# A linear-attention recurrence with two expert layers: chunks of 128 tokens cut into sub-chunks of 64 on 64x64 matmul tiles

## The reference, cut to what matters

```
cur  = (u * k_t) outer v_t
y_t  = r_t @ (state + cur)
state = w[:, None] * state + k_t outer v_t
```

```
logits = x @ phi                       # 3072 x 32 slots, 8 experts of 4 slots
d = softmax of logits over tokens;  slot_input = d.T @ x
slot_out = relu(slot_input @ w1[e]) @ w2[e]      # 384 -> 1024 -> 384 per expert
c = softmax of logits over slots;   x2 = c @ slot_out
out = relu(x2 @ w_in) ** 2 @ w_out     # 384 -> 2048 -> 384
```

## Time and profile before

| what | us |
|---|---|
| time, median of 3 runs (465.07 to 466.24) | 465.87 |
| profiled execution, span from first to last instruction | 464.3 |
| first output of a unit ends | 23.08 |
| last output of a unit (unit 23) ends | 178.30 |
| first matmul of the experts | 190.56 |
| first matmul of the last stage | 228.05 |

### The profile page before, as it was taken

One profiled execution on the slowest core, in us unless ns is written; L12 is line 12 of the kernel. 1 busy time (PEld: TensorE's weight loads), 2 busy tenths in 40 slices (PEclk: granted clock), 3 DMA queues, 4 the chain that ended last, 5 costly groups with the idle time before them and its releaser, 6 DMA issues.

```text
span 464.3 us, 8783 instructions
## 1 busy us (share of the span) xinstructions
PE 405.0 (87%) x3096; PEld 349.0 (75%) x3096; DVE 331.9 (71%) x439; ACT 174.4 (38%) x312; POOL 153.1 (33%) x111
## 2 busy tenths in 40 slices
PE   0856968778787889999679999999999999999997
PEld 0544857657676766235279999999999999999997
DVE  8599999999999994611596565565556556556553
ACT  2011313123031314012535555555555555555552
POOL 6578878898888850110550000000000000000000
PEclk9957999999998989899889999999999999999999
DMA  6966667667666769999600010001001001001001
GB/s 174 243 195 193 202 206 218 183 201 231 194 196 203 225 238 316 373 373 403 212 0 1 1 68 2 1 1 68 0 0 68 0 0 68 0 0 68 1 0 68
DMA packets 31844, 60.30 MB, mean 130 GB/s; under 512 B 2640, under 2 KB 25296, under 8 KB 31440
## 3 DMA queue, kind: packets, MB, share of 16 engines
q1 hardware_dynamic: 31824, 60.02, 40.9%
HBM read 55.30 MB, written 4.72 MB: 129 GB/s over the span
## 4 chain that ended last, share of the span: by engine, by line
PE 61%; DVE 14%; POOL 10%; issue 5%; DVEq 1%; ACT 1%; POOLq 0%; ACTq 0%
PE out_ps L1081 43%; POOL scores L413 8%; PE h_ps L1059 5%; DVE scores L667 4%; DVE queries L644 4%; PE wide L997 3%; PE wide L1022 2%; PE score_ps L865 2%; DVE bonus L662 1%; DVE state L680 1%; PE y_ps L890 1%; POOL ruk L402 1%; POOL ruk L405 1%; PE wide L948 1%; DVE keys L638 1%
## 5 line engine op out<-in xcount | busy, mean ns | idle before, releaser
L1081 PE MATMUL out_ps<-w_hi,act_hi 128*128 128x384 f32 x384 | 130.5, 340 | 5.2 <-DVE act_lo L819 4.0
L1081 PE MATMUL out_ps<-w_hi,act_lo 128*128 128x384 f32 x384 | 131.0, 341 | 0.0
L1081 PE MATMUL out_ps<-w_lo,act_hi 128*128 128x384 f32 x384 | 130.5, 340 | 0.0
L814 DVE TENSOR_TENSOR act<-relu_h 128x512 f32<-128x512 f32 x96 | 68.2, 711 | 78.3 <-ACT relu_h L576 78.3
L576 ACT ACTIVATE relu_h<-h_ps 128x512 f32<-128x512 f32 x96 | 57.3, 597 | 100.6 <-PE h_ps L1059 97.9
L865 PE MATMUL score_ps<-queries,keys 112*128 112x256 f32 x192 | 60.5, 454 | 29.7 <-DVE queries L644 29.7
L413 POOL TENSOR_TENSOR scores<-ident,bonus 128x1024 f32<-128x1024 f32 x24 | 74.4, 3101 | 23.2 <-DVE bonus L662 23.2
L1081 PEld LDWEIGHTS out_ps<-w_hi,act_hi 128*128 128x128 f32 x384 | 72.7, 189 | 6.2 <-ACT act_hi L579 3.3
L1081 PEld LDWEIGHTS out_ps<-w_lo,act_hi 128*128 128x128 f32 x384 | 72.9, 190 | 3.8
L1081 PEld LDWEIGHTS out_ps<-w_hi,act_lo 128*128 128x128 f32 x384 | 72.5, 189 | 0.0
L819 DVE TENSOR_TENSOR act_lo<-act,act_hi 128x512 fp32r<-128x512 f32 x96 | 68.4, 713 | 4.6 <-ACT act_hi L579 1.0
(11 more groups left out here) (145 smaller groups left out, 369.1 us busy)
## 6 DMA issues: line engine op xcount, KB each, us to landing
rkv<-in_rkv_n SPq DMA_DIRECT2D x24, 576.0 KB, 4.6
rk<-in_rk_t SPq DMA_DIRECT2D x48, 192.0 KB, 3.2
w_sb<-in_w SPq DMA_DIRECT2D x24, 384.0 KB, 5.1
w_room<-in_w SPq DMA_DIRECT2D x4, 1536.0 KB, 11.1
out_dram<-y_sb SPq DMA_DIRECT2D x5, 768.0 KB, 3.5
w_x<-in_w SPq DMA_DIRECT2D x2, 1536.0 KB, 14.0
w_w<-in_w SPq DMA_DIRECT2D x4, 768.0 KB, 11.5
w_in_sb<-in_w_in SPq DMA_DIRECT2D x3, 1024.0 KB, 13.0
```

Of the source, the lines that this page charges most:

```text
L814: nc.vector.tensor_tensor(act[f % 2][:, :], relu_h[f % 2][:, :], relu_h[f % 2][:, :], ALU.mult).then_inc(act_done, 1)
L1081: last = nc.tensor.matmul(out_ps[t][:, 0:DM], a[f % 4][:, tok], w[:, f], start=(f == 0 and i == 0), stop=(f == NF - 1 and i == 2))
```

## The change

The 24 units stay, but each is cut into two sub-chunks of 64 tokens, and all matmuls of the recurrence are made of pieces with at most 64 rows and at most 64 columns of weights: `unit_scores` makes 16 matmuls of 48 rows and 128 columns, `unit_state` 16 of 64 rows and 48 columns, the output 32 of 64 columns (`within`, `from_state`), half of them before and half of the second kind after the transposes. The state is carried in two steps per unit (`state_b` after the first sub-chunk, `state_end` after the second; ScalarE scales it into `state_a`). The bonus is a second set of scores from `queries` scaled by u*w (`second_queries` on ScalarE), and of it only the diagonal is copied; GpSimd's products and its matrix of the bonus are gone. The keys with tokens on partitions are no longer loaded and scaled but turned on chip (`turn_keys`, then `copy_keys` on ScalarE), so of the natural layout only the values are loaded. GpSimd makes `keys` and `queries` (`times_keys`, `times_queries`), without the padding. x is turned per unit instead of per chunk, in `turn_x` (4 transposes). The softmax over tokens is kept running: per chunk a new maximum (`new_peaks`), the exponents (`exponents`), a turn of both logits and exponents, a `gather` of that chunk and an update of the sum `acc` (`gathered`). `w1` gets room for all 8 experts, in halves of 512 columns loaded from chunk 0 on, and `w2` of 2 experts is loaded in the recurrence as well; the other 4 of the first 6 follow at its end. Of the loops, TensorE's body now covers chunks 1 to 4, and SyncE, ScalarE and VectorE have bodies for 1 to 3 of the chunks. Order on TensorE in unit n: state n, scores n+1, first half of output n, in the first unit of a chunk the slot logits of the chunk before, turn of keys n+2, in the second unit the turned logits, turn of x n-1, in the second unit the gather, second half of output n. The stages after the gather are as before, but for addresses, and for GpSimd's selection matrices, which no longer wait for the mixing weights.

The core of the diff (the removed products of GpSimd and VectorE are in the functions above; blank lines are left out):

```diff
+SUBS = (slice(0, SUB), slice(SUB, P))
+LOGS = 6
 TILES = B * CH
 DM = H * D
 KD = DM // P
...
+            def load_rows(c, hp):
+                n = HP * c + hp
+                if isinstance(c, int) and c == 0:
+                    if hp < 2:
+                        sp.wait_ge(rk_cleared, hp + 1)
+                    else:
+                        sp.wait_ge(rk_cleared_late, 1)
+                elif isinstance(c, int) and c == 1:
+                    sp.wait_ge(k_first, hp + 1)
+                wait(sp, q_done, n - 3)
                 for half, rows in enumerate(HEAD_ROWS):
-                    sp.dma_start(phi_sb[rows, :, :], phi.rearrange("(a h d) s -> h d a s", h=2, d=D)[half]).then_inc(params_in, 16)
-            def load_unit(c, hp, first):
-                n = HP * c + hp
-                wait(sp, qk_done, n - 1)
-                if first and hp < 2:
-                    sp.wait_ge(rk_cleared, hp + 1)
-                for half, rows in enumerate(HEAD_ROWS):
-                    sp.dma_start(rk[hp % 2][rows], rk_t[c, hp, half]).then_inc(rk_in[hp % 2], 16)
-                wait(sp, y_done, n - 3)
-                wait(sp, kn_done, n - 3)
-                wait(sp, aux_done, n - 3)
-                wait(sp, rk_prod_done, n - 3)
-                sp.dma_start(rkv[hp][:, :, :, :], rkv_n[c, hp]).then_inc(rkv_in[hp], 16)
-                if first and hp == 0:
-                    load_params()
...
+            def load_vals(c, hp):
+                wait(sp, y_mm, HP * c + hp - 3)
+                sp.dma_start(vals[hp][:, :, :], rkv_n[c, hp][:, 2]).then_inc(vals_in[hp], 16)
+            def load_w1(e, half):
+                part = slice(FE // 2 * half, FE // 2 * (half + 1))
+                sp.dma_start(w1_sb[:, e, :, part], w1[e].rearrange("(k p) f -> p k f", p=P)[:, :, part]
+                             ).then_inc(w1_in, 16)
...
+            chained(nc.gpsimd.memset(swap[:, :], 0.0))
+            for rows, cols in ((slice(0, D), slice(SECOND, PAIR)), (slice(SECOND, PAIR), slice(0, D)),
+                               (slice(SECOND // 2, SECOND), slice(D, SECOND))):
+                own = slice(rows.start, rows.stop) if rows.start != SECOND // 2 else cols
+                chained(nc.gpsimd.tensor_copy(swap[rows, cols], ident[rows, own]))
+            def times_keys(c, hp):
                 n = HP * c + hp
-                pool.wait_ge(rkv_in[hp], 16 * (c + 1))
-                wait(pool, bonus_done, n - 1)
-                nc.gpsimd.tensor_tensor(ruk[hp % 2][:, :, :], rkv[hp][:, 0], rkv[hp][:, 1],
-                                        ALU.mult).then_inc(rk_prod_done, 1)
-                pool.wait_ge(rk_prod_done, n + 1)
-                nc.gpsimd.tensor_tensor(ruk[hp % 2][:, :, :], ruk[hp % 2][:, :, :],
-                                        u_all[:, 2 * D * hp:2 * D * (hp + 1)].unsqueeze(1).broadcast_to([P, B, 2 * D]),
-                                        ALU.mult).then_inc(ruk_done, 1)
-            def diagonal(m, hp):
-                pool.wait_ge(bonus_done, m + 1)
-                wait(pool, y_done, m - 1)
+                pool.wait_ge(rk_in[hp], 32 * (c + 1))
+                wait(pool, score_mm, n - 3)
+                nc.gpsimd.tensor_tensor(keys[hp][0:PAIR], rk[0:PAIR, hp, 1],
+                                        powers[0:PAIR, 1, hp, 1:P + 1].unsqueeze(1).broadcast_to([PAIR, B, P]),
+                                        ALU.mult).then_inc(k_done, 1)
+            def times_queries(c, hp):
+                n = HP * c + hp
+                pool.wait_ge(rk_in[hp], 32 * (c + 1))
+                wait(pool, y_mm, n - 3)
                 nc.gpsimd.tensor_tensor(
-                    scores[hp % 2][:, :, :, :].rearrange("p b h t -> p (b h) t"),
-                    ident[:, :].unsqueeze(1).broadcast_to([P, 2 * B, P]),
-                    bonus[hp % 2][:, :, :].rearrange("p b h -> p (b h)").unsqueeze(2).broadcast_to([P, 2 * B, P]),
-                    ALU.mult).then_inc(diag_done, 1)
...
+            def copy_ya(n, hp):
+                sc.wait_ge(y_mm, n + 1)
+                nc.scalar.activation(x_t[0:PAIR, hp, :, 0:SUB],
+                                     y_ps[0:PAIR, 0:B * SUB].rearrange("p (b t) -> p b t", t=SUB),
+                                     ACT.Copy).then_inc(ya_done, 1)
+            def second_queries(c, hp):
+                n = HP * c + hp
+                sc.wait_ge(q_done, n + 1)
+                wait(sc, score_mm, n - 1)
+                if isinstance(c, int) and c == 0:
+                    sc.wait_ge(uw_done, 1)
+                nc.scalar.activation(queries[0:PAIR, 2, hp % 2], queries[0:PAIR, hp // 2, hp % 2],
+                                     ACT.Copy, scale=uw[0:PAIR, hp:hp + 1]).then_inc(q2_done, 1)
+            def carry(c, hp):
+                sc.wait_ge(end_done, HP * c + hp + 1)
+                nc.scalar.activation(state_a[0:PAIR, hp], state_end[hp % 2][0:PAIR], ACT.Copy,
+                                     scale=w_128[0:PAIR, hp:hp + 1]).then_inc(a_done, 1)
+            def copy_keys(c, hp):
+                n = HP * c + hp
+                sc.wait_ge(kt_mm, n + 1)
+                wait(sc, inc_mm, n - 1)
+                nc.scalar.activation(
+                    keys_n[hp % 2][:, :, :, :],
+                    turn_ps[:, :].rearrange("p (b h e) -> p b h e", h=2, e=SECOND)[:, :, :, 0:D],
+                    ACT.Copy).then_inc(kt_done, 1)
...
+            def exponents(c):
+                sc.wait_ge(peak_done, c + 1)
+                wait(sc, acc_done, c)
+                nc.scalar.activation(ALPHA, STEP, ACT.Exp).then_inc(alpha_done, 1)
+                nc.scalar.activation(p_sb[:, :], lg_sb[:, :], ACT.Exp, bias=NEW_PEAK).then_inc(p_done, 1)
...
+            def copy_yb(n, hp):
+                ve.wait_ge(y_mm, n + 1)
+                nc.vector.tensor_copy(x_t[0:PAIR, hp, :, SUB:P],
+                                      y_ps[0:PAIR, BANK:BANK + B * SUB].rearrange("p (b t) -> p b t", t=SUB)
+                                      ).then_inc(yb_done, 1)
...
+                ve.wait_ge(inc_mm, n + 1)
+                inc = [inc_ps[0:PAIR, BANK * j:BANK * j + SPARE].rearrange("p (b d) -> p b d", d=D) for j in range(2)]
                 if isinstance(c, int) and c == 0:
...
+                    nc.vector.tensor_copy(state_b[0:PAIR], inc[0]).then_inc(b_done, 1)
+                else:
+                    ve.wait_ge(a_done, n - HP + 1)
+                    nc.vector.tensor_tensor(state_b[0:PAIR], inc[0], state_a[0:PAIR, hp], ALU.add).then_inc(b_done, 1)
+                if isinstance(c, int) and c == CH - 1:
+                    return
+                ve.wait_ge(b_done, n + 1)
+                wait(ve, a_done, n - 1)
+                nc.vector.tensor_tensor(state_end[hp % 2][0:PAIR], inc[1], state_b[0:PAIR], ALU.add).then_inc(end_done, 1)
...
-            def mask_scores(hp):
-                nc.vector.copy_predicated(scores[hp % 2][:, :, :, :].rearrange("p b h t -> p (b h) t"),
-                                          mask[:, :].unsqueeze(1).broadcast_to([P, 2 * B, P]),
-                                          score_ps[hp % 2][:, :].rearrange("p (a t) -> p a t", t=P)
-                                          ).then_inc(mask_done, 1)
...
+                wait(ve, y_mm, n - 1)
+                parts = score_ps[:, :].rearrange("p (a k t) -> p a k t", k=2, t=SUB)
+                into = scores[hp % 2][:, :, :, :].rearrange("p h b t -> p (h b) t")
+                nc.vector.copy_predicated(into, strict[:, :].unsqueeze(1).broadcast_to([P, 2 * B, SUB]), parts[:, :, 0]
+                                          ).then_inc(mask_half, 1)
+                ve.wait_ge(const_step, MASKS)
+                ve.wait_ge(mask_half, n + 1)
+                nc.vector.copy_predicated(into, diag[:, :].unsqueeze(1).broadcast_to([P, 2 * B, SUB]), parts[:, :, 1]
+                                          ).then_inc(masked, 1)
+            def new_peaks(c):
+                ve.wait_ge(lg_done, c + 1)
+                wait(ve, p_done, c)
+                nc.vector.reduce_max(PEAK, lg_sb[:, :], AX.X).then_inc(peak_step, 1)
+                ve.wait_ge(peak_step, 3 * c + 1)
+                nc.vector.scalar_tensor_tensor(NEW_PEAK, PEAK, -1.0, OLD_PEAK, ALU.mult, ALU.min).then_inc(peak_step, 1)
+                ve.wait_ge(peak_step, 3 * c + 2)
+                nc.vector.tensor_tensor(STEP, NEW_PEAK, OLD_PEAK, ALU.subtract).then_inc(peak_step, 1)
+                ve.wait_ge(peak_step, 3 * c + 3)
+                nc.vector.tensor_copy(OLD_PEAK, NEW_PEAK).then_inc(peak_done, 1)
+            def gathered(c, parts):
+                ve.wait_ge(alpha_done, c + 1)
+                ve.wait_ge(gather_mm, c + 1)
+                for cols, part in zip((slice(0, XHALF), slice(XHALF, XC)), parts):
+                    last = nc.vector.scalar_tensor_tensor(acc[:, cols], acc[:, cols], ALPHA, part, ALU.mult, ALU.add)
+                last.then_inc(acc_done, 1)
...
+            def turn_keys(c, hp):
```

(93 more changed lines are left out.)

842 lines of the change are left out of this document (396 added, 446 removed).

## The result

The changed kernel takes 421.6 us (median of 4 runs, 418.7 to 428.3), the kernel before 466.1 (4 runs beside it): ratio 0.902, interval 0.898 to 0.907. Forecast were 401.1 us and 386 to 441. The profiled span is 420.2 us against 464.3. Timed again it took 422.1 us, ratio 0.901 (0.896 to 0.907). Ratios leave out runs that took over 1.5% more than the fastest of the same kernel, and the profiled runs of experiments 5, 6, 7 and 9 are such longer ones.

The account below looks back on a forecast made before the run. The prediction took shared SBUF access between VectorE and GpSimd, and the chain through it, as the bound. Start 17 + 23 x 4.4 + tail 45.05 + last stage 236.25 = 399.5 us span, plus 1.6: 401.1 us; range 386 to 441.

Parts of the forecast that it names:

- row halves: Rival, TensorE: matmuls in different row halves don't run together, so a unit takes 6.1 us, total 440.2; chance 0.14.
- code: Rival, TensorE: larger loop body doesn't stay on chip, three further passes reload it, up to 58 us, total 459; chance 0.07.
- The unit: Steady recurrence unit, set by TensorE: 3.32 us work, 0.40 tile-shape changes, 0.33 waits, 0.35 for short records: 4.4 us.
- holds: VectorE's maximum steps and sum update each hold TensorE some 0.6 us in a chunk's first and second units: 0.33 a unit.
- short records: TensorE may not issue many short matmul records at full speed; 0.35 us a unit allowed, between nothing and 0.87.
- Four pieces at once: TensorE: four independent 64x64 pieces run together, giving 3.32 us of work a unit; two at once would give 5.44.
- Records as the limit: Rival, TensorE: at 22 ns a record the unit takes 4.9 us, total 412.6; chance 0.16.
- The start: Time to the first output: first scores at half clock, masks 1.6 us, some 2 us after; 17 us, between 15 and 20.
- the 23 units at one price: Recurrence after the first output: all 23 units at 4.4 us each, last output near 118 us.
- The rival of half clock: TensorE granted 1.2 GHz in the recurrence: 7.37 us a unit, total 469.4, slower than before; chance 0.06.
- Tail and last stage: After the last output: 45.05 us of tail, experts starting 7.5 us in, then an untouched last stage of 236.25 us.
- All products with two SBUF operands leave: VectorE in the steady loop: these products go, ending mutual waiting with GpSimd; VectorE takes 2.9 to 3.2 us a unit.

Follow-up runs that it names:

- experiment 5: The changed kernel unaltered, run again beside other variants; 422.1 us (417.4 to 424.4).
- experiment 6: The changed kernel with some 50 unread matmuls on zeros keeping TensorE busy before its first transposes, between them and before the second scores; 433.4 us, ratio 0.921.
- experiment 7: The changed kernel with expert weights loaded later: w1 from chunk 2 on, four pieces of w2 behind the recurrence; 419.9 us, ratio 0.899.
- experiment 9: The changed kernel with a short warm start of 12, 6 and 5 filler matmuls on TensorE; 426.4 us, ratio 0.907.
- experiment 4: The kernel before, with GpSimd's three operations per unit cut to a corner and the bonus left out elsewhere; 440.6 us, ratio 0.941.
- experiment 2: The changed kernel with all w1 and the early w2 expert weights loaded after the recurrence's loads; 430.6 us, ratio 0.920.
- experiment 8: The changed kernel with GpSimd making each key product twice from chunk 1 on; 425.5 us, ratio 0.914.
- experiment 1: The changed kernel with each unit's 16 score matmuls reordered, all of the first head, then all of the second; 421.1 and 433.9 us.
- experiment 11: The changed kernel with two one-column steps of the running maximum taking the old maximum as a scalar operand; 424.8 us, ratio 0.908.
- experiment 10: The changed kernel with both the short filler warm start and the expert weights loaded later; 421.3 us, ratio 0.902.
- experiment 12: The changed kernel with the old maximum as scalar operand and the expert weights loaded later; 424.6 us, ratio 0.908.

## Why the prediction was right, and what it missed

**The number: in part luck.** 421.6 us lies outside the forecast's own 389 to 414. It lies in 386 to 441 because that range was stretched over the rivals of row halves and of code. Row halves do run together, and code cost time in another way than the rival had it.

**The direction and its reasons: right.** VectorE and GpSimd did wait for each other (experiment 4: 1.49 to 0.69 us and 1.04 to 0.42), and with VectorE's two-operand products gone TensorE became the bound. Experiment 2 shows that DMA doesn't set the unit, experiment 8 that GpSimd doesn't, and experiment 1 that time added on TensorE adds to the unit in full.

**The unit: right.** 4.27 us against 4.4. TensorE is busy 15.55 / 4 = 3.89 of it and idle 0.38; the sum had 3.32 + 0.40 and holds of 0.33, so 0.2 of the 0.35 for short records was needed. The idle time only looks like the forecast's: of the two holds a chunk one came, 0.63 us, and the rest is the 0.74 us at the turn of the loop. TensorE idling there was named as a sign that the prediction is wrong; it came true, at 0.2 us a unit. VectorE 2.97 (2.9 to 3.2), ScalarE 2.39 (2.6), GpSimd 2.35 (2.4 to 2.7).

**Four pieces at once: right.** The 32 score records start within 0.83 us; the eight steps were put at 0.88. By this the Trainium skill's four independent tiles (TensorEngine Tiling (Array Packing), Available Configurations) hold here.

**Records as the limit: wrong here.** The 32 records of the state start within 0.35 to 0.37 us, 11 to 12 ns apart, with the 0.36 forecast. The least of 25 ns between starts that the Trainium skill gives (TensorE: Matmul & The Clock Gate, Wait — 56ns, not 53.3ns?) is not seen between these records on separate tiles.

**The start: 3.1 us short.** The sum had the first scores at half speed, the masks, and "some 2 us" for what follows. It left out the scores of unit 1, which TensorE makes ahead of the first output (15.60 to 17.58 us), and all on that path goes at half speed, not the first scores alone. Experiment 9 has the start at full speed and its first output at 17.1, where 17 was forecast with the first scores at half speed: an agreement by chance.

**The step that failed: the 23 units at one price.** 23 x 4.4 = 101.2 stood in the sum; they took 121.3. At the steady 4.27 they would take 98.2, so 23.1 us are not steady. Stops on issue sum to 17.8 us; 2.1 of them are the turns of the loop, which the 4.27 already holds, so 15.6 count. The wait behind the slow small steps is 1.7. The rest, 5.8, is by subtraction; the 23.9 us at the lower clock can account for it, which no run shows by itself. Code was in the forecast only as a rival, "three further passes are loaded again"; that doesn't happen. What costs is the first pass of any code, and chunks 0, 1 and 5 all run once or for the first time. Unrolling puts the price at 10.2 us a chunk: five packets of 2.0 us, where the rival had six pieces at nothing to 3.2. The rival of half clock had the size about right: 6.85 us a unit in experiment 1, where it had 7.37 for a steady one; but those were units of chunk 0, which have fewer products, in an order whose scores take 0.8 us longer at that speed, so the agreement is rough. It was wrong as to the place: in the changed kernel half speed comes at the start and after stops, and goes again.

**Tail and last stage: right within 1 to 2 us.** From last output to last stage 44.1 us (45.05), the experts 8.5 us after the last output (7.5), the last stage 234.7 (236.25). The sum by its own steps: 399.5 + 3.1 + 20.1 - 0.9 - 1.6 = 420.2.

**"All products with two SBUF operands leave": not quite.** The column steps L756 and L758 stayed, and cost 2 us when they met GpSimd. The Trainium skill (SBUF — State Buffer, SBUF: two separate sides) says that a VectorE instruction with two SBUF inputs and a GpSimd instruction that reads SBUF shut each other out for its whole length; the earlier trace rows, experiment 4 and the slow steps of 106.47 and 107.48 us agree, down to a single column, and in experiment 11, with the second input as a scalar operand, they did not shut each other out.

**Left open:** why stops of the same code differ from run to run. With the weights gone or later they sum to less before 75 us in each of four pairs of profiles: 7.6 against 13.8 (experiment 2 and the changed kernel), 7.1 against 11.5 (7 and 5), 10.2 against 12.7 (10 and 9), 10.7 against 15.5 (12 and 11), and unit 8 comes 5.7 to 11.5 us earlier. But with the same loads and the same TensorE code they range from 9.4 (experiment 8) to 15.5 us (experiment 11). The time at the lower clock between units 0 and 8 varies as much, from 6.8 us in experiment 2 to 34.1 in 9 and 11, and wasn't varied by itself. A version with less TensorE code outside the loop wasn't tried.

## What to carry to other kernels

Count the matmul instructions that run for the first time, outside a loop or in its first pass, apart from the steady unit, and price each 16 KB of them (here 2.0 us, with weights loading beside it); smaller tiles make more of them. When a change makes the steady unit right to 3% and the total wrong by 20 us, look at where the outputs come, one by one, before doubting the unit. And give a VectorE step beside busy GpSimd one tensor and a scalar operand, even for a single column.

## What the hardware showed that was not expected

- The granted clock reads 1.00 from 17 to 47 us in experiment 1 while the transposes start 0.2 us apart instead of 0.115. The trace holds no record of the clock before 51.2 us there, and the row reads 1.00 until the first one. Before it, spacings of like instructions tell the level.
- TensorE was busy without a pause from 17 us on in experiment 1, and its spacings were those of the lower level until 50 us; in experiment 6 fillers from 4.32 us on were at the higher one by 7.2 us.
- Every stop on issue of over 1 us in the recurrence, 76 in twelve profiles, ended 1.2 to 1.8 us after the end of a 16 KB packet of code.
- In experiment 1 TensorE, at the lower level until 50 us, never waited for code up to then, and unit 8 came at 73 us as in the changed kernel. In experiments 9 and 11 it did wait at that level, 1.1 to 2.5 us at a time.
- Records on separate 64 x 64 tiles start 11 to 12 ns apart on average. And with the two row halves issued one after the other, the second half's records start while the first half's are still under way (0.5 us after the first).
- A step on a 128 x 1 operand takes 0.16 us, or up to 1.22 beside a GpSimd product; as tensor with scalar operand it took 0.21 in all 24 cases, four of them beside a product.
